# Low parts of weights by adding transfers, tile 0's attention ahead of the next preparation, output by channels, moved sums

## What is computed

```python
def _attn_ref(q, k, v, a_re, a_im):            # B, H, S, D = 4, 8, 768, 48
    mag = np.sqrt(a_re * a_re + a_im * a_im)
    scale = np.minimum(mag, 0.999) / (mag + 1e-06)
    a_re_n, a_im_n = (a_re * scale, a_im * scale)
    for t in range(S):                         # the state is complex, D x D per head
        new_re = ar * S_re - ai * S_im
        new_im = ar * S_im + ai * S_re
        S_re, S_im = (new_re + kv, new_im)     # kv: outer product of k[t] and v[t]
        y[:, :, t] = np.einsum('bhd,bhde->bhe', q[:, :, t], S_re)

def reference(**kwargs):
    x = attention output as (B * S, H * D)     # 3072 tokens, 384 channels
    h = x @ w_in                               # 384 -> 2048
    x = (np.maximum(h, 0.0) + np.log1p(np.exp(-np.abs(h)))) @ w_out      # 2048 -> 384
    a = x @ w1; b = x @ w2                     # 384 -> 1024 each
    return ((a * b) @ w3) @ w_out2             # 1024 -> 1024 -> 384
```

## Time and profile before

| | us |
|---|---|
| median of 3 runs | 1001.27 (998.71 to 1001.32) |
| the profiled execution | 1001.37, its span 999.6 |
| PE busy | 908.0 (91% of the span) |
| DVE busy | 608.2 (61%) |
| ACT busy | 428.4 (43%) |
| POOL busy | 70.3 (7%) |

### The profile page before, as it was taken

One profiled execution on the slowest core, in us unless ns is written; L12 is line 12 of the kernel. 1 busy time (PEld: TensorE's weight loads), 2 busy tenths in 40 slices (PEclk: granted clock), 3 DMA queues, 4 the chain that ended last, 5 costly groups with the idle time before them and its releaser, 6 DMA issues.

```text
span 999.6 us, 14524 instructions
## 1 busy us (share of the span) xinstructions
PE 908.0 (91%) x5442; PEld 827.3 (83%) x5442; DVE 608.2 (61%) x974; ACT 428.4 (43%) x618; POOL 70.3 (7%) x56
## 2 busy tenths in 40 slices
PE   0963839999999999999899999998999999999998
PEld 0533739889989889899899999998888888888887
DVE  5978878989898898899889732355221212121211
ACT  3152263575574674664664654586102020202011
POOL 0000000000000000000000000000222222222221
PEclk9995668999999999999999999999999999999999
DMA  9666066273372380570570540421101010101000
GB/s 336 234 192 187 20 189 131 74 182 102 106 175 78 121 214 25 151 193 13 154 193 13 145 106 13 148 86 46 33 1 64 1 64 1 63 0 63 0 32 32
DMA packets 98663, 99.52 MB, mean 100 GB/s; under 512 B 6944, under 2 KB 91936, under 8 KB 98592
## 3 DMA queue, kind: packets, MB, share of 16 engines
q1 hardware_dynamic: 98592, 98.59, 34.4%
HBM read 63.96 MB, written 29.88 MB: 94 GB/s over the span
## 4 chain that ended last, share of the span: by engine, by line
PE 64%; DVE 22%; DVEq 6%; issue 3%; ACT 3%; DMA 2%; ACTq 0%; SPq 0%
PE ps_p L1312 8%; PE ps_p L1314 8%; PE ps_p L1313 8%; PE ps L1312 4%; PE ps L1314 4%; PE ps L1313 4%; PE ps_ay L1348 3%; PE ps L1509 3%; PE ps L1507 3%; PE ps L1508 3%; DVE sp L1191 2%; PE ps_ay L1313 2%; PE ps_ay L1314 2%; DVE an L1018 2%; PE ps_ay L1312 2%
## 5 line engine op out<-in xcount | busy, mean ns | idle before, releaser
L646 POOL TENSOR_TENSOR abl<-ab,abh 128x512 fp32r<-128x512 f32 x48 | 69.4, 1445 | 922.5 <-DVE abh L1295 922.5
L1312 PE MATMUL ps_p<-x1h,win_h 128*128 128x384 f32 x336 | 118.3, 352 | 16.9 <-DVE sp L1191 16.9
L1312 PE MATMUL ps<-g_h,wo_h 128*128 128x384 f32 x384 | 132.7, 346 | 0.0
L1314 PE MATMUL ps<-g_h,wo_l 128*128 128x384 f32 x384 | 129.6, 337 | 0.0
L1313 PE MATMUL ps<-g_l,wo_h 128*128 128x384 f32 x384 | 129.3, 337 | 0.0
L1314 PE MATMUL ps_p<-x1h,win_l 128*128 128x384 f32 x336 | 113.9, 339 | 0.0
L1313 PE MATMUL ps_p<-x1l,win_h 128*128 128x384 f32 x336 | 113.7, 338 | 0.0
L1348 PE MATMUL ps_ay<-stq,stk 96*128 96x128 f32 x384 | 56.7, 295 | 35.8 <-DMA vt<-in_v 12.8
L1286 DVE TENSOR_TENSOR ab<-ps_ay,bc 128x512 f32<-128x512 f32 x24 | 16.6, 693 | 117.0 <-ACT bc L914 117.0
L762 ACT ACTIVATE g_h<-sp 128x768 fp32r<-128x768 f32 (+1 forms) x71 | 55.5, 781 | 74.2 <-DVE sp L1191 74.2
L1348 PEld LDWEIGHTS ps_ay<-stq,stk 96*128 96x128 f32 x384 | 54.1, 208 | 37.1 <-issue 24.0
(11 more groups left out here) (167 smaller groups left out, 2050.9 us busy)
## 6 DMA issues: line engine op xcount, KB each, us to landing
qk_scr<-tt SPq DMA_DIRECT2D x16, 576.0 KB, 4.7
stq<-qk_scr SPq DMA_DIRECT2D x48, 192.0 KB, 4.8
qk_scr<-pp SPq DMA_DIRECT2D x16, 576.0 KB, 4.2
stk<-qk_scr SPq DMA_DIRECT2D x48, 192.0 KB, 4.5
an<-in_a_re SPq DMA_DIRECT2D x8, 576.0 KB, 4.0
...
```

What stands on the lines that cost most here:

```text
L646: tensor_tensor(abl[:, m % AR, :], ab[:, m % 2, :], abh[:, m % AR, :].bitcast(F32), ALU.subtract).then_inc(ab_lo, 1)
L1312: mm(o, wh, xh, start=start, stop=False)
L1314: return mm(o, wl, xh, start=False, stop=stop)
```

## The change

1. *Low parts of w_in and w_out.* DVE's `raw_low` is gone. ACT copies each piece twice: rounded, into the high part, and rounded with the sign turned, into the low part. Then GpSimd's queue re-reads the piece from DRAM and adds it there in place (`accum_op=ALU.add`), in 28 transfers. The `raw` buffer is free when ACT is done. `up(0, 0)` waits for the 12 of w_in, `down(0, 0)` for the 16 of w_out. The last four pieces are handled on ACT between the groups of tile 0's attention.
2. *Tile 0's attention* comes ahead of tile 1's first run; tile 1's preparation goes on between the groups and ends behind them.
3. *Slot 0* is written out by itself (`first_slot`): tile 1's attention stands at steps 2 to 7, not 0 to 5, with tile 2's preparation; the last `down` of tile 0 stays in it.
4. *Sums.* q is made in two halves, the second behind the sum of step 4, and the keys of step 5 come behind the sum. So in all slots that prepare.
5. *Output by channels.* `down2` takes w34 as weights and streams 512 tokens, three groups of 128 channels; the result is stored channel by channel.

```diff
@@ SP
             def store_q(m, first=False):
-                wait(prep_q, m + 1)
                 if not first:
                     for c in range(NCH):
                         wait(q_rd[c], 32 * m)
                 for i in range(2):
+                    wait(prep_q, 2 * m + i + 1)
                     eng.dma_start(c_p(qk_scr[i]), by_g(tt[:, i, :])).then_inc(q_wr, 16)
@@ GpSimd
+            for i in range(8):
+                eng.wait_ge(raw_hi, i + 1)
+                for g in range(G if i < 4 else 4):
+                    eng.dma_start(piece_to[i][1][:, g, :], piece_src[i][:, g, :].bitcast(F32R), accum_op=ALU.add)\
+                        .then_inc(win_lo if i < 4 else wo_lo, 16)
@@ ScalarE
-                act(piece_to[i][0], piece(i), ACT.Copy).then_inc(raw_hi, 1)
+                act(piece_to[i][0], piece(i), ACT.Copy)
+                act(piece_to[i][1], piece(i), ACT.Copy, scale=-1.0).then_inc(raw_hi, 1)
...
             for i in range(NG):
                 if i + 1 < NG:
                     k_by_tokens(0, i + 1)
+                if i < 4:
+                    raw_high(4 + i)
                 y_out(0, i, first=True)
...
+            def first_slot():
+                for j in range(NP1 - 1):
+                    if j >= 3:
+                        y_out(1, j - 3)
+                    def between():
+                        if j == 6:
+                            prep_psquare(2, 0)
+                        if j >= 2:
+                            k_by_tokens(1, j - 2)
+                    softplus(0, j + 1, False, between)
+                    if j == 1:
+                        prep_log(2)
+                        prep_root(2)
+                    if j == 6:
+                        prep_psquare(2, 1)
+                    g_high(0, j + 1, False)
+                    if j == 0:
+                        prep_squares(2)
+                    if j == 1:
+                        prep_root_square(2)
+                y_out(1, 4)
+                prep_inverse(2)
+                y_loaded(1, 0)
+                x1_high(1, 0)
+                y_out(1, 5)
+                prep_squares(3)
+                y_loaded(1, 1)
+                x1_high(1, 1)
+                prep_log(3)
+                prep_rsqrt(3)
+                softplus(1, 0, False)
+                g_high(1, 0, False)
@@ VectorE
-            after_mask = {0: steps("run", 1), 1: steps("run", 5), 2: steps("carry", 2), 3: by[:2], 4: ["q"], 5: ["inverse", "keys"]}
-            after_sum = {0: steps("run", 2), 1: steps("run", 6), 2: steps("carry", 4), 3: by[2:3], 4: ["p2"], 5: []}
+            after_mask = {0: steps("run", 1), 1: steps("run", 5), 2: steps("carry", 2), 3: by[:2], 4: [("q", 0)], 5: ["inverse"]}
+            after_sum = {0: steps("run", 2), 1: steps("run", 6), 2: steps("carry", 4), 3: by[2:3], 4: [("q", 1), "p2"], 5: ["keys"]}
...
+            def first_slot():
+                for j in range(NP1 - 1):
+                    if j >= 3:
+                        new_state(1, j - 3)
+                    if j >= 2:
+                        prep(2, True, first_before_mask[j - 2])
+                        mask_scores(1, j - 2)
+                        prep(2, True, after_mask[j - 2])
+                    add_relu(0, j + 1, False)
+                    if j >= 2:
+                        prep(2, True, after_sum[j - 2])
+                    g_low(0, j + 1, False)
+                    if j == 0:
+                        prep(2, True, ["m2"])
+                    if j == 1:
+                        prep(2, True, ["newton", "scale start", "scale"])
+                mask_scores(1, 5)
+                prep(2, True, ["inverse", "keys", "keys end"])
+                x1_low(1)
+                prep(3, False, ["m2", "newton", "scale start"])
+                add_relu(1, 0, False)
+                prep(3, False, ["scale"] + steps("a", 0))
+                g_low(1, 0, False)
@@ TensorE
-            eng.wait_ge(raw_lo, 8)
+            eng.wait_ge(win_lo, 16 * 4 * G)
...
             up(0, 0)
-            slot(0, True, True, prev=False)
+            for j in range(NP1):
+                if j < NP1 - 1:
+                    up(0, j + 1)
+                if j >= 2:
+                    scores(1, j - 2)
+                if j == 0:
+                    eng.wait_ge(wo_lo, 16 * 4 * 4)
+                down(0, j, False)
+                if j >= 2:
+                    outputs(1, j - 2, False)
+            up(1, 0)
+            slot(1, True, False, prev=False)
...
-                for s_ in range(4):
+                for mo in range(G):
...
-                    mm(ps_o[s_], ah, w34h[:, m, :], start=m == 0, stop=False)
-                    mm(ps_o[s_], ah, w34l[:, m, :], start=False, stop=False)
-                    last = mm(ps_o[s_], al, w34h[:, m, :], start=False, stop=m == NM2 - 1)
+                    last = mm3(ps_o[mo], w34h[:, m, ms], w34l[:, m, ms], abh[:, m % AR, :], abl[:, m % AR, :],
+                               m == 0, m == NM2 - 1)
```

More of the change, by code:

```diff
@@ L764, in _ @@
             prep_squares(0)
-            raw_high(0)
             prep_log(0)
             prep_rsqrt(0, first=True)
-            raw_high(1)
-            raw_high(2)
-            raw_high(3)
+            for i in range(4):
+                raw_high(i)
             prep_psquares(0)
@@ L777, in _ @@
                 w34_rows(mi)
-            for i in range(4, 7):
-                raw_high(i)
             k_by_tokens(0, 0)
@@ L1075, in prep @@
                         prep_p_(m, even, first)
-                    elif piece == "q":
-                        prep_q_(m)
+                    elif piece[0] == "q":
+                        prep_q_(m, piece[1])
                     elif piece == "p2":
@@ L1150, in _ @@
             tokens_mask()
[L1151 to L1159 removed]
+            prep(0, True, ["m2", "newton", "scale start", "scale"] + steps("a", 0, 1) + steps("run", 1, 2, 3, 4, 5, 6, 7) +
+                 ["ends"] + steps("carry", 1, 2, 4, 8, 16, 32) + by +
+                 ["p", ("q", 0), ("q", 1), "p2", "inverse", "keys", "keys end"], first=True)
             prep(1, False, ["m2", "newton", "scale start", "scale"] + steps("a", 0, 1))
[L1161 to L1164 removed]
             mask_scores(0, 0)
[L1166 to L1167 removed]
+            between = [steps("run", 1), steps("run", 2), steps("run", 3), steps("run", 4), steps("run", 5), steps("run", 6),
+                       steps("run", 7) + ["ends"], steps("carry", 1), steps("carry", 2, 4), steps("carry", 8),
+                       steps("carry", 16, 32), by[:1]]
             for i in range(NG):
@@ L1173, in _ @@
                 prep(1, False, between[2 * i + 1])
-                if i == 2:
-                    raw_low(7)
-            prep(1, False, ["q"])
+            prep(1, False, by[1:])
             x1_low(0)
-            prep(1, False, ["p2", "inverse", "keys", "keys end"])
-            prep(2, True, ["m2"])
+            prep(1, False, ["p", ("q", 0), "p2", ("q", 1), "inverse"])
             def low_x2_first(times):
@@ L1201, in _ @@
             add_relu(0, 0, False)
-            prep(2, True, ["newton", "scale start", "scale"] + steps("a", 0))
+            prep(1, False, ["keys"])
             g_low(0, 0, False)
+            prep(1, False, ["keys end"])
             def slot(n, att, has_prep, nxt_prep, even, nxt=True, weights=False):
```

91 lines of the change are left out of this document (34 added, 57 removed).

## The result

The changed kernel takes 1034.4 us in the median (1032.8 to 1038.5, 4 runs) against 1001.0 of the kernel before (998.7 to 1001.3, 4 runs): 1.0345 times the time before, 95% interval 1.0311 to 1.0379. The profiled execution of the changed kernel is its slowest (1038.5, span 1036.3), 4.1 us above the median.

The account below looks back on a forecast made before the run. PE's own columns were taken to bound the kernel from 227.6 us on, with lower clock and waits winnable earlier. From 1001.4, parts 1 to 3 gave -3.5, moved sums -6, output by channels -2: 990 us, range 984 to 997.

Parts of the forecast that it names:

- 28 transfers on the GpSimd queue ... I take 2: Low parts of w_in and w_out: each adding transfer takes 2 us (bounds 1.1 to 4.4), w_out's sixteen done at 114.
- The upper bound of 152: Latest forecast end, in us, of w_out's sixteen additions, started at 82 and taking 4.4 us each.
- their stacks land 9.8 later as before: Tile 0's preparation: stacked keys land 9.8 us after the keys are ready at 62.5, so at 72.3.
- E: End of tile 0's attention on PE: 124.93 before, forecast 107 (bounds 101 and 114), 18 us earlier.
- 11.1 us of PE waiting: Before tile 0's first mask: PE's wait while VectorE did four runs and three subtractions, from 80.97 to 92.08.
- Mask to E is 31: Tile 0's attention: 31 us from first mask to E (bounds 26 and 34), for 32.9 before.
- the walk: Step-by-step forecast of slot 0 after E: down(1, 0) at E + 117 instead of E + 102.5, 14.5 us given back.
- The net of parts 1 to 3: Up to down(1, 0): 18 us won at E less 14.5 lost in slot 0, so -3.5 (bounds -14 and +6).
- C: Rival: w_out's additions gate down(0, 0); total 1001.4 at 3.6 us each, 1014 at 4.4 (24 late); chance 0.13.
- 4.4 is for four times the bytes: Argument against C: the 4.4 us transfer time was read from a whole piece, with four times an addition's bytes.
- B: Rival, all given back: slot 0's transitions cost 6 more, moved sums give 2 instead of 6; about 1000; chance 0.17.
- A: Rival: the head start keeps more, E 5 us earlier and half-clock stretches 5 us shorter; about 980; chance 0.20.

Follow-up runs that it names:

- e9_parts45: The kernel before with only the moved sums and the output by channels, all else as before: 987.7 us, ratio 0.9876.
- e5_low_only: e9_parts45 plus low parts by GpSimd additions, one PE wait per piece, attention and slot 0 ordered as before: 978.4 us, ratio 0.9795.
- e1_staged: The changed kernel with a semaphore and PE wait for each weight piece, instead of one wait for all additions of w_in or w_out: 994.4 us, ratio 0.9953.
- e2_dve_low: The changed kernel with low parts subtracted on VectorE again and no transfers on GpSimd's queue: 1000.2 us, ratio 1.0005.
- e6_scratch: The changed kernel with 1024 instead of 512 bytes for GpSimd's descriptors, tiles moved up 512 bytes: 997.5 us.
- e7_plain: The changed kernel with w_out's sixteen transfers as plain copies without addition (output wrong), w_in's twelve still adding: 996.0 us.
- e11_pause: e1_staged with 1024 descriptor bytes and GpSimd holding back from piece 2 until tile 0's key stores landed: 993.1 us, ratio 0.9946.
- e3_out_channels: The kernel before with output by channels alone, 9 matmuls of 512 columns for 12 of 384: 994.1 us, ratio 0.9940.

## Why the prediction was wrong, point by point

**The four steps from before to after.** They follow from the ratios, in us of 1000:

| step | from, to | us |
|---|---|---|
| parts 4 and 5 | before, e9_parts45 | -12.4 |
| additions, one wait a piece, order of before | e9_parts45, e5_low_only | -8.1 |
| parts 2 and 3 | e5_low_only, e1_staged | +15.8 |
| one wait for all of w_out | e1_staged, changed | +39.2 |

The sum is +34.5, the result. With the subtractions on VectorE instead, parts 2 and 3 cost 12.9 (e9_parts45, e2_dve_low). By the spans of the profiled executions the third step is 14.1, so it is known to about 2 us.

**1. Low parts.** The failed step is "28 transfers on the GpSimd queue ... I take 2", with its bounds. Three of its terms were off. *Each:* 5.2 us for w_out's, 6.6 for w_in's. *The start:* at 2 us each I had w_in's done at 41 and so counted w_out's from 82, when I had ACT's copy. But the same queue holds both in order, and w_in's took until 96; and ACT's copies, behind the attention's first, let the first addition go at 88.7 even where the queue was free (e6_scratch). The upper bound of 152 took the price of 4.4 and kept the start at 82. That goes together, since twelve at 4.4 from 17.6 end at 70; but twelve at the measured 6.6 end at 96. So of the 26 us from 152 to 178, 14.5 are the start and 11.5 the price. *The assumption under both:* that a transfer on its own queue overlaps the next. It does where the descriptors have room (e6_scratch), and the 512 bytes stand in the last lines of both kernels, where I gave them no weight. The estimate by the Trainium skill's page "DMA: Bandwidth & Descriptors", section "Anatomy of one DMA — SWDGE (gpsimd) path" (2.0 us plus bytes over 436 GB/s, 2.45 us for 192 KB) does not agree for additions, 3.5 us at the least and 3.8 in the median to landing with hardly any other traffic; the plain copies of e7_plain, 2.7 and 3.1, come nearer. The keys of tile 0 were ready at 63.0 (60.50 + 2.56) for 62.5. But "their stacks land 9.8 later as before" failed: 14.1 in e1_staged, since the stores of the keys, now beside the additions, take 9.2 us for the 5.4 of before, and the stacks wait for them on SyncE. In the profiled execution of the changed kernel it is 19.2, but up to there e1_staged issues the same, so those further 5 are of that execution (e7_plain, also the same up to there, has its stacks at 77.2). PE's product started at 25.13, not 28.

**2. Attention ahead.** Mask 79.8 in e1_staged for 76; E 109.3 for 107, inside its bounds, and the -18 is nearly there (-15.6). The failed step is whose it is. I counted "11.1 us of PE waiting" as what part 2 takes away, but of the subtractions, seven lie ahead of the first mask before, and part 1 alone brings that mask to 81.8 and E to 112.2 (e5_low_only). Part 2 by itself is worth 2.9 at E, all of which x1's low parts take back: 7.85 us to `up(0, 0)` for 4.97. e11_pause shows besides that a mask at 76.8 does not give E 107: the clock came back later by what the start was earlier. "Mask to E is 31" was 29.5 there and 33.5 here.

**3. Slot 0.** Each landmark of the walk is right within 2 us. E to `down(1, 0)` was forecast as 117 and is 117.1 in e1_staged; `down(0, 0)` starts 22.0 behind E (21 forecast), `outputs(1, 0)` waits 4.37 (4.5), `up(1, 0)` comes 103.6 behind E (102). The net of parts 1 to 3 at `down(1, 0)` is -1.0 for -3.5, inside the bounds; but it holds what part 4 gives in slot 0, and slot 1 loses 1.8 us more up to `up(2, 0)`. Against e9_parts45, which has parts 4 and 5 alone, e1_staged is +2.4 at `down(1, 0)`, +4.0 at `up(2, 0)`, and +7.7 by the ratios: parts 1 to 3 are a loss even with one wait a piece. The net hid a bad part beside a good one: against e5_low_only, which has part 1 and not the other two, e1_staged is 12.4 later at `down(1, 0)` (226.45 for 214.01) and 14.0 at `up(2, 0)`.

**4. Moved sums.** -7.0 for -6, but from other places: slots 1 to 5 gave 3.1 to 4.0, slot 0 2.0 to 3.4. That the number is near is luck. The waits fell from 16.9 to 4.9, under the 8 forecast; not every us of wait taken away came back as time.

**5. Output by channels.** Direction right, size mis-sized: -5.4 for -2, outside its bounds. The term was the difference of two nearly equal products, 2.10 and 2.05 us a step; with the measured 2.105 and 2.04 it is 3.1 us. And a term was put at nothing: `up2`, unedited, gave 2.0 (e3_out_channels).

**The rivals.** C was the right one: same place, same mechanism, `down(0, 0)` waiting for w_out's last addition. It had 0.13, and its worst price was 24 us late (1014 us) for the 39.2 of the runs. "4.4 is for four times the bytes" was the argument against it, and bytes were not what set the time. B was right in kind about parts 2 and 3, and nothing showed A. Without the gate the number would have held, 994.4 in the forecast's range of 984 to 997, but in part by luck: parts 4 and 5 gave 12.4 us for the 8 of the sum, and parts 1 to 3 cost 7.7 where the sum has a gain of 3.5 and its bound is a loss of 6.
